# A pooled-attention and two-layer-pair kernel whose tokens go through in four units of 864 in place of six of 576

## What is computed

```python
k_p = k.reshape(B, H, S // 8, 8, D).mean(axis=3)          # v_p likewise
attn = softmax(scale * q @ k_p.T);  x = attn @ v_p        # B=H=8, S=576, D=64
h = x @ w_in;  g = s * maximum(h, 0)**2 + b;  x = g @ w_out      # 4608 tokens, 512 -> 2048 -> 512
h = x @ w2_in; g = h * sigmoid(h);            out = g @ w2_out
```

## Time and profile before

| | |
|---|---|
| runs | 1690.76 us median of 3 (1683.76 to 1696.36) |
| profiled execution | 1693.99 us, its span 1692.2 us |
| granted TensorE clock, mean | 0.982 of full |
| PE busy | 1614.3 us, 95% of the span |
| DVE busy | 1073.7 us, 63% |
| ACT busy | 927.5 us, 55% |
| POOL busy | 239.5 us, 14% |
| SP's transfer queue | 531.43 MB, 87.2% of 16 engines' span |
| granule loads | 784 of 512 KB |

### The profile page before, as it was taken

The page is one execution under the profiler, slowest core; times in us unless marked ns, Lnnn a source line. Parts: engine busy times, 40 slices in busy tenths (PEclk is TensorE's granted clock), DMA queues, the critical chain, the costliest instruction groups (busy, mean ns, idle before and its releaser), DMA issues.

```text
span 1692.2 us, 29600 instructions
## 1 busy us (share of the span) xinstructions
PE 1614.3 (95%) x11926; PEld 1600.0 (95%) x11926; DVE 1073.7 (63%) x1309; ACT 927.5 (55%) x1286; POOL 239.5 (14%) x294
## 2 busy tenths in 40 slices
PE   7988997899999999999999999999999999999999
PEld 6988997899999999999999999999999999999998
DVE  6686677376574757557575674837657475654645
ACT  4574554565547555574555645556454755547443
POOL 5320220120201112011120201112011120000000
PEclk9999999999999999999999999999999999999999
DMA  6789787989898998989889898998989899899997
GB/s 191 278 321 346 297 313 291 394 295 326 300 374 306 340 322 301 378 307 332 303 317 376 298 339 306 359 350 299 325 295 384 307 333 316 272 391 330 331 327 259
DMA packets 155222, 542.75 MB, mean 321 GB/s; under 512 B 16592, under 2 KB 16592, under 8 KB 153040
## 3 DMA queue, kind: packets, MB, share of 16 engines
q1 hardware_dynamic: 150736, 531.43, 87.2%
q10 hardware_dynamic: 4352, 9.44, 1.4%
HBM read 464.39 MB, written 76.41 MB: 320 GB/s over the span
## 4 chain that ended last, share of the span: by engine, by line
PE 76%; DMA 10%; DVE 8%; ACT 3%; issue 2%; SPq 0%; DVEq 0%; ACTq 0%
PE a_ps L745 20%; PE a_ps L767 20%; PE b_ps L767 15%; PE b_ps L745 13%; DMA xa_dram<-probs 6%; PE a_ps L671 2%; DMA w_raw<-weights 2%; PE t_ps L625 2%; PE t_ps L638 2%; DMA ring<-w_dram 2%; DVE w_sum L1156 2%; DVE ring L1141 1%; PE t_ps L611 1%; ACT ring L840 1%; DVE gq L1200 1%
## 5 line engine op out<-in xcount | busy, mean ns | idle before, releaser
L745 PE MATMUL a_ps<-xc_hi,ring 128*128 128x288 f32 x1792 | 404.5, 304 | 20.2 <-DVE gq L1200 15.7
L767 PE MATMUL a_ps<-sp_hi,ring 128*128 128x288 f32 x1792 | 368.7, 295 | 1.4 <-DMA ring<-w_dram 1.4
L745 PEld LDWEIGHTS a_ps<-xc_hi,ring 128*128 128x128 f32 x1792 | 306.7, 193 | 24.0 <-DVE gq L1200 17.7
L745 PE MATMUL b_ps<-xc_hi,ring 128*128 128x288 f32 x1344 | 302.4, 300 | 13.7 <-DVE gq L1200 13.6
L767 PEld LDWEIGHTS a_ps<-sp_hi,ring 128*128 128x128 f32 x1792 | 291.2, 188 | 1.9 <-DMA ring<-w_dram 1.9
L1241 DVE TENSOR_TENSOR sp_lo<-gq,sp_hi 128x1152 fp32r<-128x1152 f32 (+1 forms) x182 | 198.1, 1101 | 132.5 <-ACT sp_hi L937 131.7
L767 PE MATMUL b_ps<-sp_hi,ring 128*128 128x288 f32 x1344 | 277.8, 295 | 0.6 <-DMA ring<-w_dram 0.6
L745 PE MATMUL a_ps<-xc_lo,ring 128*128 128x288 f32 x896 | 269.4, 301 | 0.0
L767 PE MATMUL a_ps<-sp_lo,ring 128*128 128x288 f32 x896 | 264.5, 295 | 0.0
L745 PEld LDWEIGHTS b_ps<-xc_hi,ring 128*128 128x128 f32 x1344 | 228.5, 191 | 15.3 <-DVE gq L1200 15.0
L937 ACT ACTIVATE sp_hi<-gq 128x1152 fp32r<-128x1152 f32 (+1 forms) x182 | 168.2, 940 | 126.5 <-PE b_ps L767 63.4
(11 more groups left out here) (168 smaller groups left out, 2570.6 us busy)
## 6 DMA issues: line engine op xcount, KB each, us to landing
ring<-w_dram SPq DMA_DIRECT2D x784, 512.0 KB, 5.6
w_dram<-w_stage SPq DMA_DIRECT2D x32, 1024.0 KB, 6.5
w_dram<-ring SPq DMA_DIRECT2D x48, 512.0 KB, 3.9
w_raw<-weights SPq DMA_DIRECT2D x16, 1024.0 KB, 6.4
out<-yb ACTq DMA_DIRECT2D x16, 576.0 KB, 7.2
k_stage<-kT SPq DMA_DIRECT2D x30, 288.0 KB, 5.7
q_sb<-qT SPq DMA_DIRECT2D x30, 288.0 KB, 6.0
v_stage<-vP SPq DMA_DIRECT2D x30, 288.0 KB
```

What stands on the lines that cost most here:

```text
L745: last = nc.tensor.matmul(bank[:, half, 0:th], w, xc_of(x, th)[:, j, k, :], start=(first and k == 0 and i == 0), stop=(k == 1 and i == 2), ...
L767: last = nc.tensor.matmul(bank[:, m, 0:th], w, split_of(g, th, turn, 2 * c + half), start=(first and half == 0 and i == 0), stop=(end and ...
```

## The change

`HALVES` becomes one unit of 2 x 288 tokens and four of 2 x 432, so the main part has 10 phases in place of 14; the first stage stays at 576 tokens. A slot of a wide phase still has 12 matmuls, now of 432 columns. The weights are loaded 10 times in place of 14 (560 granules for 784). To make room, `ring` has 6 granules in place of 8, `xr` is gone (the next unit's x is loaded into the part of `gq` that holds block 3, block 22 in matrix terms, once its last user is done, and the load stands seven slots later), and `w_raw`, `w_sum` and `w_stage` of the first stage lie over the ends of `gq`, `xc_hi`, `xc_lo`, `sp_hi` and `sp_lo`, which the first stage and unit 0, with 288 columns, leave free. With six granules the second half of a set's plain parts is prepared at slot 6 of the set before and not at slot 2. Since there are fewer units, the jobs are placed anew: six in the first stage in place of four, six in each of units 0, 1 and 2, four in unit 3; before there were four in each of units 0 to 5.

```diff
-HALVES = (288,) * 7
+HALVES = (288,) + (432,) * 4
-XR_SLOTS = (11, 13, 15, 17, 19, 21, 23)
-RING = 8
+XR_SLOTS = (15, 17, 19, 21, 23, 25, 27)
+RING = 6
-FIRST_TURNS = ((0, SPACED), (17, SPACED), (64, SPACED), (81, SPACED))
 TIGHT = (0, 1, 2, 3, 4, 6, 7, 8, 9, 11, 12, 13, 14)
-TURN_SLOTS = ((0, SPACED), (17, OVER_EDGE), (SLOTS, TIGHT), (SLOTS + 15, TIGHT))
+CLOSE = tuple(range(13))
+FIRST_UP = 3
+FIRST_TURNS = tuple((layer * 64 + 13 * n, CLOSE) for layer in range(2) for n in range(FIRST_UP))
+SIX = tuple((15 * n, TIGHT) for n in range(6))
+FOUR = ((0, SPACED), (17, OVER_EDGE), (SLOTS, TIGHT), (SLOTS + 15, TIGHT))
+UNIT_TURNS = (FIRST_TURNS, SIX, SIX, SIX, FOUR)
...
-        xr = sb("xr", [P, KC * 2 * TM])
+        def x_of(ph):
+            s, layer = divmod(ph, 2)
+            if layer:
+                return yb[:, :]
+            at = 24 * HALVES[s - 1] if s else G_FIRST
+            return gq[:, at:at + 2 * KC * HALVES[s]]
...
             def load_x(s):
                 if s:
-                    sp.wait_ge(xlo_ready, (2 * s - 1) * NPROD)
+                    sp.wait_ge(dlo_ready, (2 * s - 1) * SPLITS + PIECE_END[7])
                 sp.wait_ge(x_stored, (batches_for(s) - 1) * PAIRS * DMA)
...
-                    if layer and slot == SLOTS_UP + RING + 3 and s + 1 < UNITS:
+                    if layer and slot == SLOTS_UP + RING + 10 and s + 1 < UNITS:
                         load_x(s + 1)
...
             def part_up(ph, g, j):
                 th = HALVES[ph // 2]
+                if ph % 2 == 0 and g == 0 and j == 0:
+                    act.wait_ge(xlo_ready, (ph + 1) * NPROD)
...
-                if i in (0, 2) and q + 1 < SETS:
-                    prep_plain(q + 1, i // 2)
+                if i in (0, 6) and q + 1 < SETS:
+                    prep_plain(q + 1, i // 6)
```

More of the change, by code:

```diff
@@ L108 @@
 OVER_EDGE = (0, 1, 2, 3, 4, 6, 7, 8, 9, 11, 12, 14, 15)
-FIRST_TURNS = ((0, SPACED), (17, SPACED), (64, SPACED), (81, SPACED))
 TIGHT = (0, 1, 2, 3, 4, 6, 7, 8, 9, 11, 12, 13, 14)
-TURN_SLOTS = ((0, SPACED), (17, OVER_EDGE), (SLOTS, TIGHT), (SLOTS + 15, TIGHT))
+CLOSE = tuple(range(13))
[4 more added lines that the diff above has]
+UNIT_TURNS = (FIRST_TURNS, SIX, SIX, SIX, FOUR)
 def schedule():
     table, t = {}, PAIRS
[L117 to L121, removed]
+    for s, slots in enumerate(UNIT_TURNS, -1):
+        for base, offsets in slots:
             for i, name in zip(offsets, TURN_NAMES):
-                table[s, base + i] = (name, job)
-        t = upto
+                assert (s, base + i) not in table
+                table[s, base + i] = (name, t)
+            t += 1
+        assert t >= batches_for(s + 1) * PAIRS
     assert t == JOBS
@@ L362, in plain_split, with ring_stored @@
         def plain_split(q, n):
-            return n + 1 if q == 0 else 4 * q - 2 + n + 1
+            return n + 1 if q == 0 else 4 * q - 2 + 2 * n + 1
         def sum_split(q, n):
-            return 4 * q + (4 if q < SETS - 1 else 2) + n + 1
+            return 4 * q + 2 + (2 * n + 2 if q < SETS - 1 else n + 1)
+        def ring_stored(granule):
+            stored = [n for n in range(granule % RING, granule + 1, RING) if n % 4 != 2]
+            assert granule % 4 != 2
+            return r_stored[granule % RING], len(stored) * DMA
         def set_stored(q, j):
@@ L465, in load_gran @@
                 else:
-                    sp.wait_ge(f_done, (SETS - 2 + n // 4) * PLAIN + PLAIN)
-                    if n % 4 != 2:
-                        sp.wait_ge(r_stored[n], SETS // 2 * DMA)
+                    last = max(g for g in range(4 * SETS) if g % RING == n)
+                    sp.wait_ge(f_done, last // 4 * PLAIN + PLAIN)
+                    sp.wait_ge(*ring_stored(max(g for g in range(4 * SETS) if g % RING == n and g % 4 != 2)))
                 sp.dma_start(ring[:, n % RING, :].bitcast(F32), w_dram[row_of(ph, slot)]
@@ L1144, in sum_set @@
             def sum_set(q, n):
-                a11, a12, a21, a22 = [w_raw[:, q % 2, i, :] for i in range(4)]
+                a11, a12, a21, a22 = [w_raw[q % 2][:, i, :] for i in range(4)]
                 s1, s2 = w_sum[:, 0, :], w_sum[:, 1, :]
@@ L1249, in xsum @@
             def xsum(ph, op):
-                src = xr if ph % 2 == 0 else yb
+                src = x_of(ph)
                 x, y, z, w = [quad(src, HALVES[ph // 2], i) for i in range(4)]
```

73 lines of the change are left out of this document (41 added, 32 removed).

## The result

The changed kernel takes 1743.65 us (median of 4 runs, 1740.21 to 1749.65), the kernel before 1691.7 us beside it: a ratio of 1.0316, 95% interval [1.0267, 1.0365]. It is slower by 3.2%, and lies above the forecast's range of 1640 to 1718 us. The profiled execution took 1745.0 us, its span is 1743.2.

What follows compares the result with a forecast made beforehand. PE, 95% busy, was taken to set the time. Matmuls -35, x load +3, main-part jobs -6, first-stage jobs +26, end +1 make -11 us: 1683 against the profiled run, about 1681 on the median's scale, range 1640 to 1718.

Steps and rivals of the forecast that it cites:

- Jobs in the main part: Units after the first stage: waits and lowered clock of the jobs, 50 us against 56, -6 us (-30 to +20).
- the x load: Unit 0: unit 1's larger x delays the granule of slot 44, +3 us (0 to 5); hidden in wide units.
- the upper bound: Main part: the slowest case for the jobs' waits and clock loss, +20 us.
- The dense jobs bind DVE: Rival, main part and first stage: both job terms at their worst, +14 and +26 us, 1721 us; chance 0.08.
- The period: Wide product matmuls: 13 ns fixed per matmul beside the columns, 193.0 ns each at 432 columns, -35 us.
- the rival of the growing price: Every wide matmul: the extra 13 ns grow with columns, period above about 198 ns, 1709 us; chance 0.20.
- that of the hidden loading: Rival, wide matmuls: weight loading is hidden, period falls to 182.5 ns, 56 us less, 1625 us; chance 0.10.
- The first stage: Slots before unit 0: three jobs a layer for two, 13 us a layer, +26 us (+12 to +40).
- my upper reckoning: First stage, worst case by turns: 6.4 us wait at turn0 for each of two handovers a layer, some 20 us a layer.
- the stall behind sub: Kernel before, 12 phases with jobs: sub waits for the last x transfer, PE waits, clock drops; 4.7 us each, 56 us.
- Sub behind the x store: Wide phases: sub's wait nearly goes, x landing about 1.7 slots after add1 where it took 3.5.
- The end: Last store of y is 864 KB, not 576: +1 us.

Runs made afterwards that it cites:

- spreading the batch: Changed kernel with slot 51's operations spread over slots 51 to 54 (DVE's seven over 52 to 54): 1711.73 us, ratio 1.0114.
- The narrow experiment: Two runs on the kernel before: six jobs in each of units 0 to 3, 1790.84 us; or six close jobs in the first stage, 1714.97 us.
- the new placement: Changed kernel with a unit's six jobs spread over other slots: 1676.64 us with slot 51 spread and own x buffer, 1709.96 us alone.
- both edits: Changed kernel with slot 51's seven DVE operations spread over slots 52 to 54 and a separate buffer for a job's x: 1699.68 us, ratio 1.0047.
- The series: Kernel before plus seven series of 144 unused matmuls behind its last product, 256 to 512 columns, weights loaded each time: 132.8 ns at 288, 195.4 at 432.
- the own buffer: Kernel before with a job's x in a place of its own from unit 0 on, over `w_raw`: 1650.46 us, ratio 0.9755.
- the own x buffer: Changed kernel with a separate buffer for a job's x, so sub does not wait for the last job's store: 1729.58 us, ratio 1.0239.

## Why the prediction was wrong

**The step that failed** is the sum of waits under *Jobs in the main part*: "unit 0 about 24 us, units 1 and 2 12 each, unit 3 [...] 2, unit 4 none: 50 against 56, -6 us". With the 3 us of the x load, which it keeps apart, it is 53; the profile has 46.2, 29.6, 31.9 and nothing, 107.7 us against 56.2: +52 instead of -3. It lies beyond the upper bound too (+20). This term alone turns a forecast of 1683 into 1738.

What went wrong in it is not the place that I had looked at, but the handovers that I had priced at nothing in the wide units, and at 3 us in unit 0. Unit 1 has 21.7 us of idle time where my terms make 10.2, and 7.9 us of lowered clock where I had 1.8. The wait for lo0 at slot 53 was put at 6.3 us in unit 0 and 8.3 in units 1 and 2, each with 1.8 of clock; the starts of matmuls there lie 7.04, 9.07 and 9.05 us apart, and spreading the batch gave 32 us. I had priced the handovers at slots 30 and 53 and taken the others to fit between, though the same reasoning holds for each: turn0 at slot 36 behind norm, values1 at 43 behind add0, scores at 45 behind add1 stand in the down half, where DVE has low parts and differences in every slot. Phase 2 has 2.1 to 2.8 us of idle time at each, 10.1 us at the four small waits, where I had 1.9 for one. The narrow experiment shows that it is not a matter of width, and the new placement that it is one of places: with both edits made, placing the jobs anew takes 23 us off (1699.7 to 1676.6), alone 34 (1743.7 to 1710.0). I had let the wide slots stretch DVE's room by 1.45, which was right where the turns are far apart (unit 3) and no help where six jobs leave no slot free. The rival *The dense jobs bind DVE* named the mechanism, with a chance of 0.08 and a price of +26 in the main part, less than half of the +55 that came. DVE was busy for 59% of unit 0 and 60% of unit 1: on the average it had time, and what came late came late by its order.

The terms were also added loosely. Those given for unit 0 (6.3 + 1.8, 1.6, two of 4.2, 3) make 21 us and not 24, and the wait at slot 53 there, 6.9 + 0.75 - 1.6, is 6.1 and not 6.3; neither changes the forecast by more than 3 us.

**The period** went the way I had taken, with a size off. Predicted 193.0 ns and -35 us; measured 195.1 in the phases: 8 x 131.1 = 1048.8 us for 1072.8, -24. The series say that a fixed price is right, 12.8 to 13.6 ns at four widths, and that 432 columns carry 2 ns more; the rival of the growing price (above 198) and that of the hidden loading (182.5) both fall. That the price is a quarter of the weight loading, as I had read it, no run shows. The Trainium skill (TensorE: Matmul & The Clock Gate, Back-to-back issue gap) has N / 2.4 + 2.5 ns for an isolated matmul, 182.5 ns at 432 columns; the series, in fp32r with weights loaded for each matmul, lie 10 to 17 ns above this formula, 12.9 at 432.

**The first stage** came near its forecast by luck, with two errors that cancel. Unit 0 was to begin 26 + 6.8 = 33 us later and began 29.5 later. The crowding alone costs 31, not 26 (the narrow experiment), and the later preparation, which I had at nothing ("its cover is thin only where DVE is late"), gives 8 back there, 15 in the kernel before. The 15 are clear: four profiles with the old preparation begin unit 0 at 295.2 to 298.9 us, three with the later one at 278.4 to 283.4. The 8 are not: the changed kernel and the two runs on it with the same first stage begin it at 325.8 to 334.1, and 336.3 is one profile. I had asked only whether the new place is late for its reader, not what leaves the old place. The waits for norm before turn0 are 3.7 to 4.8 us at each of the four handovers, below the 6.4 of my upper reckoning; the scores' waits of 3.1 and 3.2 us for add1 I had not priced.

**The ring and x.** Wide phases hide the ring of six, as said: the trace names no wait for a granule in units 1 to 3. In unit 0 I had 3 us for the x load; the distance of starts at slot 44 of its second phase is 2.59 us for a usual 0.13. "I am wrong if [...] granules of the shorter ring are waited for all through unit 0" did not happen. In a kernel of narrow units alone the ring of six costs 27 us.

**What the kernel before lost.** I had put all of its 56 us on the stall behind sub; the own buffer takes 43 of them away.

**Sub behind the x store.** That its wait nearly goes in wide phases held (unit 3 loses nothing; the own x buffer gives nothing in unit 1). **The end** and the jobs' PE work are as in the sum.

The sum with the measured terms, against the span of 1692.2: -24 for the matmuls, +51.5 for the losses of the units, +29.5 for the first stage, -6.8 for two jobs' work that moved there, +1 for the end: +51, and the span is 51.0 us longer.

## What to carry to other kernels

When a change packs the same small work into fewer units, price each handover of the packed order, not the two that look worst: list, for each turn that PE waits for, what stands ahead of it in the strict order of the engine that makes it. A neighbour without the crowding (unit 3 here) and the crowding without the rest of the change (the narrow run) tell which of them pays. Before buying time with bigger tiles, take the stall that the profile already names: an own buffer for one staged result and a preparation moved by four slots gave 3.4% together, where the wide matmuls gave 24 us, 1.4%. The fastest wide kernel measured here has both of these too and takes 1676.64 us; the fastest narrow one takes 1632.17. A wide kernel with four jobs in the first stage and fewer than six in a unit was not run.

## What the runs showed of the hardware

- A matmul in fp32r with its weights loaded each time took 12.8 to 13.6 ns above its columns at 2.4 GHz for 256, 288, 384 and 512 columns, but 15.4 at 432 and 19.9 at 448, with all other engines idle (one execution, 144 matmuls a width). The best width of these per column is 512 (0.443 ns a column; 0.452 at 384 and 432, 0.461 at 288 and 448).
- Idle time of PE cost more than itself. In unit 0 of the changed kernel PE is idle for 245.4 - 217.2 = 28.2 us, and its busy time is 217.2 - 199.2 = 18.0 us over what it is at full clock (granted 0.93). With the stall behind sub gone from the kernel before, the granted clock of phase 2 rose from 0.98 to 1.00.
